# First attention in 32- and 64-row tiles on one Trainium2 core: row sums from a column of ones, division after the values

## The reference

```
attention: 8 heads of 64 channels, scores = q k^T / 8
  heads 0-3: query i sees keys i-31 .. i             (local)
  heads 4-7: query i sees keys j <= i with i % 32 == j % 32   (strided)
  attn = exp(scores - max) / (sum + 1e-9);  out = attn @ v
mixing: theta = x @ w_theta; zr, zi = x cos(theta), x sin(theta)
  y = w_tok_r @ zr + w_tok_i @ zi;  u = x + y;  u + relu(u @ w_ch)
experts: gate = softmax of the 2 largest of x @ w_gate (4 experts)
  each expert: causal attention with head size 64, times its gate, @ wo, summed
```

## Time and profile before

| | us |
|---|---|
| median of 3 runs | 575.8 |
| profiled execution, its own time | 575.45 |
| its span, first to last instruction | 573.7 |
| PE busy | 545.1 |
| DVE busy | 348.9 |
| ACT busy | 259.6 |

### The profile page before, as it was taken

How to read it: one execution, slowest core, us unless ns; L and a number is a source line. 1 busy time by engine, 2 the same in 40 slices (tenths; PEclk the granted TensorE clock), 3 DMA queues, 4 the chain that set the end, 5 groups by cost and what they waited for, 6 DMA issues and landing times.

```text
span 573.7 us, 11679 instructions
## 1 busy us (share of the span) xinstructions
PE 545.1 (95%) x4473; PEld 467.0 (81%) x4473; DVE 348.9 (61%) x843; ACT 259.6 (45%) x775; POOL 130.4 (23%) x131
## 2 busy tenths in 40 slices
PE   6999999999999999999999999999999999999986
PEld 5777889989866799899876689999976679998764
DVE  1677856675888622476678741567677952343683
ACT  2874734555533541355553542255643454121453
POOL 4550710022221250011321152011131126000110
PEclk9999999999999999999999999999999999999999
DMA  9742046221000114211000012331000010000002
GB/s 224 178 115 77 1 112 158 67 49 27 2 0 1 38 47 112 66 43 30 14 1 2 19 65 55 83 83 23 22 1 1 1 75 10 1 2 1 0 1 83
DMA packets 73413, 27.13 MB, mean 47 GB/s; under 512 B 68624, under 2 KB 68624, under 8 KB 73360
## 3 DMA queue, kind: packets, MB, share of 16 engines
q1 hardware_dynamic: 68848, 24.38, 16.7%
q10 hardware_dynamic: 4512, 2.02, 1.3%
HBM read 21.67 MB, written 4.72 MB: 46 GB/s over the span
## 4 chain that ended last, share of the span: by engine, by line
PE 74%; DVE 15%; ACT 5%; issue 3%; POOL 2%; POOLq 0%; DVEq 0%; ACTq 0%
PE acc L1278 33%; PE wide L1278 14%; PE wide L1350 4%; PE turned L1447 4%; PE turned L1391 3%; PE wide L1371 3%; PE turned L1404 2%; DVE xt L1106 2%; PE turned L1421 2%; DVE nmax L1049 2%; PE turned L1489 2%; PE turned L1311 2%; ACT probs L902 2%; PE wide L1335 1%; DVE probs L1080 1%
## 5 line engine op out<-in xcount | busy, mean ns | idle before, releaser
L814 POOL TENSOR_TENSOR probs<-probs,rec 96x768 f32<-96x768 f32 (+1 forms) x16 | 21.7, 1354 | 204.2 <-DVE rec L1064 204.2
L910 ACT ACTIVATE pt<-turned 128x384 f32<-128x384 f32 (+3 forms) x64 | 30.8, 481 | 77.4 <-PE turned L1404 41.4
L895 ACT ACTIVATE probs<-wide,nmax 96x128 f32<-96x128 f32 (+1 forms) x176 | 61.5, 369 | 9.0 <-DVE nmax L1045 8.9
L823 POOL TENSOR_TENSOR probs<-probs,weight 128x128 f32<-128x128 f32 (+4 forms) x36 | 26.9, 767 | 145.9 <-DVE weight L1087 145.9
L902 ACT ACTIVATE probs<-wide,nmax 128x128 f32<-128x128 f32 (+4 forms) x72 | 39.0, 553 | 36.2 <-DVE nmax L1049 25.6
L1278 PE MATMUL wide<-w_tok_hi,z_hi 128*128 128x288 f32 x216 | 47.4, 300 | 0.0
L1278 PE MATMUL wide<-w_tok_hi,z_lo 128*128 128x288 f32 x216 | 46.0, 293 | 0.0
L1278 PE MATMUL wide<-w_tok_lo,z_hi 128*128 128x288 f32 x216 | 45.9, 293 | 0.0
L1049 DVE TENSOR_REDUCE nmax<-wide 128x1 f32<-128x128 f32 (+4 forms) x72 | 33.1, 512 | 13.1 <-PE wide L1376 13.0
L840 POOL TENSOR_TENSOR z_lo<-absf,z_hi 128x512 fp32r<-128x512 f32 x20 | 26.3, 1317 | 63.9 <-ACT z_hi L958 63.9
L1278 PE MATMUL acc<-xu_hi,w_ch_hi 128*128 128x288 f32 x128 | 39.3, 307 | 1.0 <-DVE xu_lo L1176 0.9
(11 more groups left out here) (190 smaller groups left out, 1458.9 us busy)
## 6 DMA issues: line engine op xcount, KB each, us to landing
raw_q<-in_q SPq DMA_DIRECT2D x32, 128.0 KB, 2.4
out<-o_sb SPq DMA_DIRECT2D x16, 256.0 KB, 2.0
raw_k<-in_k SPq DMA_DIRECT2D x28, 128.0 KB, 2.5
raw_v<-in_v SPq DMA_DIRECT2D x64, 31.5 KB
raw_v<-in_v SPq DMA_DIRECT2D x14, 120.0 KB
raw_r<-in_moe_w_tok_r SPq DMA_DIRECT2D x1, 1152.0 KB, 6.3
stage<-in_moe_w_theta ACTq DMA_DIRECT2D x2, 512.0 KB, 7.5
raw_i<-in_moe_w_tok_i SPq DMA_DIRECT2D x1, 1024.0 KB, 7.9
```

The lines of the kernel that those rows point to most:

```text
L814: g.tensor_tensor(pr, pr, rec[0:rows, 1, 0:nt].unsqueeze(2).broadcast_to([rows, nt, w]), ALU.mult).then_inc(s["probs_pool"], 1)
L823: ins = g.tensor_tensor(pr, pr, weight[:, j:j + 1].broadcast_to([P, n]), ALU.mult)
L895: e = a.activation(probs[0:rows, hh, t * P:t * P + w], wide[slot][0:rows, t * P:t * P + w], ACT.Exp, bias=nmax[0:rows, hh, t:t + 1], accum ...
L910: ins = a.activation(dst, src, ACT.Copy)
```

## The change

The first attention (s1) is computed in small tiles. A local unit has 18 tiles of 32 queries by 64 keys (the 32 own keys and the 32 before them), a strided unit has 10 tiles of 3 classes (54 rows) and one of 2 (36). Four tiles of 32 rows, or two of 64, lie under each other on the partitions of PSUM, so one unit's scores fill one buffer of `wide`: one bank a head, 5 columns of 64 keys (local) or 6 (strided). The masks become one bf16 product a head; a small product with `never` closes the 32 keys before the first query.

The exponentials keep their number nearly (10 or 12 of 64 columns, in place of 12 or 10 of 126 and 128) and make no sums. One transpose takes both heads of a column (5 or 6 in place of 12 or 10). In `values` the transposed probabilities are the stationary operand, and v moves, with a column of ones added (65 columns): the result has queries on partitions, its 65th column is the row's sum. `norm` reads the sums there, and divides while it copies to `x_tok`. A new step `back` transposes `x_tok` (5 or 6 transposes) and `xt` is copied from that. POOL has no part in s1's `norm` any more; ACT makes the copies of both q and k. v is loaded in other pieces (6 DMAs a unit; for local heads each row twice), the masks are built after the semaphore that lets PE begin, and six products that nobody reads ("fill") stand first on PE.

`PROLOGUE` and `BODY` are now written out as lists of steps, in another order, s3, theta and out included. `EPILOGUE` is the same. The diff, cut to its core, with one line of the new lists:

```diff
-LQ = 96
-L_T = S // LQ
+W = 64
+L_T = S // STRIDE
 R_N = S // STRIDE
-R_T = P // R_N
+R_T = W // R_N
 SQ = R_T * R_N
 S_T = (STRIDE + R_T - 1) // R_T
-S_LAST = S - SQ * (S_T - 1)
+COLS = (S_T * W + P - 1) // P
+ZONE_A = 2 * (2 * NT + 6) * 2 * D + 2 * S + 36
+PROBS = 6 * P
+DV = D + 1
 MASKED = -1.0e30
...
+    ("exp", "s3", 0, 1, 1), ("scores", "s3", 1, 0), ("theta", 1, 0, 2), ("norm", "s3", 0, 1, 1), ("done", "theta", 0),
...
+    if k == "back":
+        return ["turned"] * 2
+    if k == "values" and step[1] == "s1":
+        return ["turned"] * 2 if step[4:] else ["wide"]
-        return ["wide"] * 2
+        return ["wide"] * (1 if step[1] == "s1" else 2)
...
-            return (LQ, L_T, P) if local(p) else (SQ, S_T, SQ)
+            return (STRIDE, L_T, STRIDE, L_T * STRIDE // P + 1) if local(p) else (W, S_T, SQ, COLS)
+        def parts(p):
+            return (0, 3), (3, tiles(p)[3])
+        def values_in(step, uses):
+            if step[4:]:
+                return [("turned", u, turned[u[0]]) for u in uses]
+            return [("wide", uses[0], wide[uses[0][0]][:, hh * 512:(hh + 1) * 512]) for hh in range(2)]
+        def place_of(uses, hh):
+            return uses[min(hh, len(uses) - 1)]
...
+            for hh in range(2):
+                if local(p):
+                    before_, own_ = [slice(hh * W + x * STRIDE, hh * W + (x + 1) * STRIDE) for x in range(2)]
+                    for dst, first, n in ((raw_v[before_, slot, 0:1, 0:D], 0, 1), (raw_v[own_, slot, :, 0:D], 0, L_T),
+                                          (raw_v[before_, slot, 1:L_T, 0:D], 0, L_T - 1)):
+                        eng.dma_start(dst, one[:, hh, first:first + n * STRIDE, :]
+                                     .rearrange("a (t p) d -> (a p) t d", p=STRIDE)).then_inc(s[f"v_loaded{slot}"], 16)
+                else:
+                    of = one[:, hh, :, :].rearrange("a (j r) d -> (a j) r d", r=STRIDE)
+                    for x in range(R_T):
+                        row = hh * W + x * R_N
+                        n = (STRIDE - x + R_T - 1) // R_T
+                        eng.dma_start(raw_v[row:row + R_N, slot, 0:n, 0:D], of[:, x:STRIDE:R_T, :])\
+                            .then_inc(s[f"v_loaded{slot}"], 16)
...
+                    for dst, use, scale in ((qt, u[0], SCALE), (kt, u[1], 1.0)):
+                        dst, src = turned_qk(dst, banks[where][use[0]][:, 0:NB], step[2], 0)
+                        wait_full(act, where, use)
+                        a.activation(dst, src, ACT.Copy, scale=scale).then_inc(read[where][use[0]], 1)
...
+                        for t in range(tiles(step[2])[3]):
+                            at0 = hh * 512 + t * W
+                            e = a.activation(tiled[:, t, hh * W:(hh + 1) * W], wide[slot][:, at0:at0 + W], ACT.Exp,
+                                             bias=nmax[:, hh, t:t + 1])
...
+                        cols = tiles(step[2])[3]
+                        places = note[("values", step[2])]
+                        heads = [slice(0, 2)] if len({u for _, u, _ in places}) == 1 else [slice(0, 1), slice(1, 2)]
+                        made = []
+                        for hs in heads:
+                            place, u, bank = places[hs.start]
+                            if place == "wide":
+                                of = wide[u[0]][:, :].rearrange("p (h n) -> p h n", h=2)
+                            else:
+                                of = bank[:, :].unsqueeze(1)
+                            made.append(of[:, :, 0:cols * DV].rearrange("p h (t n) -> p h t n", n=DV))
+                            wait_full(dve, place, u)
+                            v_.tensor_scalar(den[:, hs, 0:cols].unsqueeze(3), made[-1][:, :, :, D:DV], EPS, None, ALU.add)\
+                                .then_inc(s["den"], 1)
+                        dve.wait_ge(s["den"], c.at("den", len(heads)))
+                        v_.reciprocal(rec[:, :, 0:cols], den[:, :, 0:cols]).then_inc(s["recip"], 1)
+                        dve.wait_ge(s["recip"], c.at("recip", 1))
+                        for hs, of in zip(heads, made):
+                            place, u, _ = places[hs.start]
+                            to = x_tok[:, 0:cols, :].rearrange("p t (h n) -> p h t n", h=2)[:, hs, :, :]
+                            v_.tensor_tensor(to, of[:, :, :, 0:D],
+                                             rec[:, hs, 0:cols].unsqueeze(3).broadcast_to([P, len(range(2)[hs]), cols, D]),
+                                             ALU.mult).then_inc(read[place][u[0]], 1)
...
+                    copies, mask = (copies_l, mask_l) if local(p) else (copies_s, mask_s)
+                    for hh in range(2):
+                        mm(wide[slot][:, hh * 512:hh * 512 + cols * W], copies[:, :],
+                           mask[:, :].unsqueeze(1).broadcast_to([part, cols, W]), start=True, stop=True,
...
+                        n = min(rows, S - rows * t)
+                        q0 = rows * t
+                        k0 = max(q0 - STRIDE, 0) if local(p) else q0
+                        row, at0 = part * t % P, part * t // P * W + (STRIDE if local(p) and t == 0 else 0)
+                        for hh in range(2):
                             hd = slice(hh * D, (hh + 1) * D)
-                            ins = mm(wide[slot][0:n, t * P:t * P + k1 - k0], qt[hd, rows * t:rows * t + n],
-                                     kt[hd, k0:k1], start=False, stop=True, skip_group_check=True)
-                            if t == nt - 1:
-                                ins.then_inc(full["wide"][slot], 1)
+                            ins = mm(wide[slot][row:row + n, hh * 512 + at0:hh * 512 + at0 + q0 + n - k0],
...
+                        part, nt, _, cols = tiles(step[2])
+                        for n, (ca, cb) in enumerate(((0, 3), (3, cols))):
+                            slot = free("turned", n)
+                            if n == 0:
+                                u = note[("scores", step[2])]
+                                pe.wait_ge(read["wide"][u[0]], u[1])
+                            for t in range(ca, cb):
+                                k = min(P, part * nt - t * P)
+                                ins = nc.tensor.transpose(turned[slot][:, (t - ca) * P:(t - ca) * P + k],
+                                                          tiled[0:k, t, :], ident[0:k, 0:k])
                             ins.then_inc(full["turned"][slot], 1)
                     else:
...
+                    places = values_in(step, uses)
+                    for t in range(nt):
+                        keys = W if local(p) else min(rows, S - rows * t)
+                        row, at0 = part * t % P, part * t // P * DV
+                        for hh, (place, u, bank) in enumerate(places):
+                            ins = mm(bank[row:row + part, at0:at0 + DV],
+                                     tiled_t[hh * W:hh * W + keys, part * t:part * (t + 1)],
+                                     raw_v[hh * W:hh * W + keys, p % 2, t, :], start=True, stop=True)
+                            if t == nt - 1 and (place == "turned" or hh == 1):
+                                ins.then_inc(full[place][u[0]], 1)
...
+                elif kind == "back":
+                    p = step[2]
+                    part, nt = tiles(p)[0:2]
+                    for place, u, _ in note[("values", p)]:
+                        pe.wait_ge(read[place][u[0]], u[1])
+                    for n, (ca, cb) in enumerate(parts(p)):
+                        slot = free("turned", n)
+                        for t in range(ca, cb):
+                            k = min(P, part * nt - t * P)
+                            ins = nc.tensor.transpose(turned[slot][:, (t - ca) * P:(t - ca) * P + k], x_tok[0:k, t, :],
+                                                      ident[0:k, 0:k])
+                        ins.then_inc(full["turned"][slot], 1)
...
```

More of the change, by code:

```diff
@@ L348, in events @@
         return {"negmax": 1}
+    if k == "load":
+        return {"ones": 1}
+    if k == "norm" and step[1] == "s1":
+        return {"den": 2 if step[4:] else 1, "recip": 1}
     if k == "norm":
@@ L1095, in emit @@
                 elif kind == "values" and step[1] == "s1":
+                    note[("values", step[2])] = values_in(step, uses)
+                elif kind == "back":
                     p = step[2]
@@ L1327, in emit @@
                     p = step[2]
[L1328 to L1337 removed]
+                    part, nt, rows, cols = tiles(p)
@@ new lines, in emit @@
+                    for u in note[("turned", p)]:
+                        pe.wait_ge(read["turned"][u[0]], u[1])
+                    for n in range(len(uses)):
+                        free("turned" if step[4:] else "wide", n)
+                    places = values_in(step, uses)
[8 more added lines that the diff above has]
+                                ins.then_inc(full[place][u[0]], 1)
@@ new lines, in emit @@
```

(8 more changed lines are left out.)

451 lines of the change are left out of this document (163 added, 288 removed), and 17 rows, old and new, of the table BODY.

## The result

The changed kernel takes 560.95 us (median of 4 runs, 559.95 to 562.62) against 575.68 (575.46 to 576.6): ratio 0.9744, 95% interval 0.9715 to 0.9773. The forecast was 557. Its profiled execution has a span of 559.9 us and lasted 561.68, 13.8 us shorter in span than that of before.

A forecast was written before the change was run, and what follows sets the result against it. PE was taken to bound the bodies, by its own work and 3.7 us of waits; in the prologue PE and DVE alternate. From 575.45, -8.7 (work), -6.0 (waits) and -4.0 (prologue), plus the median's offset, gave 557; range 545 to 574.

The forecast's parts named there:

- PE's work in a body, -2.9: s1 on PE in each body: 14.2 us for four units against 17.1, so -8.7 us for three bodies.
- 14 ns a pass: s1's scores and values on PE: 464 passes a body at 14.4 ns, 6.7 us; bounded by 7 and 60 ns.
- Rival 2: Scores and values on PE: eight tiles overlap, 7 ns a pass in local units; 545 us with waits going too; chance 0.11.
- Waits in the bodies, -2.0 each: PE's nine waits in a body: 2.0 of 3.7 us go, -6.0 for three; bounds 0 and -11.
- Prologue, -4: Prologue and what follows up to the first body: steps (a) to (d) taken as -4 us, bounds 0 and -8.
- so nothing, and up to +1: v's more and smaller loads, behind theta's step: values stand 8 us or more later, so nothing; up to +1 in first unit.
- Step (a): Start of the prologue: PE's first instruction waits less for POOL's mask work, -2.0 us, with 0.5 as lower bound.
- (b): Prologue, first to last scores, three loops in 24.4 us: put at 0, bounds -3 and +3.
- (c): Prologue, last scores to theta: 9.4 us in place of 10.7, so -1.3.
- (d): Behind theta: `back` and `xu` of the last quarter +0.5; the `w_tok_lo` wait goes, -1.3 with the small ones.
- the -0.8: Forecast difference for the stretch from theta to the first body, -0.8 us.
- Exponentials at 0.22: ACT: s1's 44 exponentials without sums at 0.22 us each in place of 0.34, giving 5 us back.

The follow-up runs named there:

- both swaps: Changed kernel with the bodies' s3, theta and out in the order of before: 568.91 us; kernel before with the new order of these: 573.41 us.
- the run with w_theta later: Changed kernel with v of the second unit, w_tok and the second half of w_theta all loaded later in the prologue: 560.71 us, ratio 0.9753.
- the one with sums: Changed kernel with row sums made again by s1's exponentials (accum_out), read by nobody: 560.08 us, ratio 0.9743.

## Why the prediction was right, and where it was off

- *PE's work in a body, -2.9.* Measured -3.2. By its terms: a local unit is now turn 0.7, masks and `never` 0.4, scores 0.85, values 0.91, back 0.7 (134.73 to 135.46 in the timeline), 3.6 us; a strided one 3.5; 14.2 for four units, the sum of the forecast. Inside, two sizes were off against each other, which is luck: passes with filling took 6.6 and not 7.9, turn and back at 0.13 to 0.15 a transpose 6.1 and not 4.8. And of the 3.2 in busy time only 2.1 came with the tiles in the old order; 1.1 came with the new list.
- *14 ns a pass.* Right in kind, and shown: with two tiles the gain is gone. The rule of the Trainium skill ("TensorE: Matmul & The Clock Gate", section "Wait — 56ns, not 53.3ns?") that starts never follow each other by less than about 25 ns doesn't hold for passes in different tiles; the trace has 11.8 on average over 72. The Trainium skill ("TensorEngine Tiling (Array Packing)", section "Key Properties") says that different tiles run in parallel, and the trace agrees, for eight tiles too: 11.8 with eight at hand, against 14.4 with four. Rival 2 (7 ns) happened in part: a group of 72 takes 0.85 us, between the 1.2 that 14.4 ns and 0.15 for filling give and the 0.65 of 7 ns.
- *Waits in the bodies, -2.0 each.* Measured -2.0 in the first body, as the sum of +0.7 (the tiles in the old order) and -2.7 (the new list), which the forecast hadn't kept apart; that it met the number is in part luck. The reason was half right. The new order of s3 took the waits for `pt`, shown by both swaps; that it was the theta products between turn and values is the reading of the lists. That DVE and ACT do less was not the cause: with the old order and the new tiles the waits stay. That the longer way to `xt` makes waits of its own was named in the prediction and priced at nothing; the tiles by themselves lengthen the waits (3.7 to 4.4), which the new order has to pay back first. So the forecast's shares, 2.9 for the tiles and 2.0 for the waits, aren't what the runs give: 1.4 for the tiles alone, 3.4 to 3.8 for the list on top.
- *Prologue, -4: failed.* The step is the one that took v's pieces "so nothing, and up to +1". v of the local units is read twice, 208 KB more a unit, into queues that were already full to 15 us; PE, now faster through its first two units, reached transfers that hadn't landed. Two waits of 3.7 us together, and slower products behind them, took the -2.0 of the start, the -1.3 at the end, and 1.5 more. The slower products are 1.4 us behind the wait for k (21.85 to 25.34, 3.49 us, where the run with w_theta later has 2.10 for the same steps at full clock) and 1.6 behind the wait for v (38.66 to 47.20, 8.54 for 6.95). With the 3.7 that is 6.7 of the prologue up to theta, which came 4.8 later than forecast; so, as an estimate from these rows, the loops themselves gained some 2 us where the forecast had 0. The late rise of the clock at the start is in this execution too. The bounds of this term, 0 and -8, didn't hold the +1.5 of this execution; the one with sums, with the same loads, has -1.3. Step (a) was right (first scores at 8.45 for 8.4). In (b) the first to the last scores took 26.6 for 24.4, in (c) the last scores to theta 12.2 for 9.4. In (d) the wait for `w_tok_lo` went, as forecast, but from theta to the first body PE's busy time rose by 1.1 us (51.0 to 52.2; `back` is 0.85 of it), and nothing of the -0.8 was left.
- *Exponentials at 0.22.* Right (0.216). The 5 us of ACT that it gives back had no effect on the time that the run with sums could show.
- *The total.* 557 for 560.95: the bodies gave 0.6 more than forecast, the prologue and what follows it up to the first body, 4.6 less by the medians.

Open: how much of the prologue each of bytes, number of transfers, issue order and the clock at the start holds. Fewer bytes helped at one place and the total by 2.8 us of median, with intervals that overlap.

## What to carry to other kernels

Small products are cheap only while neighbours in the instruction stream lie in different tiles of the array: write the loops so that output group and head change from one product to the next, and price them by a row with as many tiles. A change that makes one stage faster should be checked against the transfers that feed it, and each transfer that is read again against how full the queues are there, by the DMA share of that stretch. Order and tile shape are one choice: the tiles alone gave 1.4 of the 5.1 us a body that both gave together. And before two prologues are compared, look where the clock of each is first recorded: two executions with the same loads were 1.6 us apart by 14 us for that alone.

## What the runs showed of the hardware

- fp32 passes of 64 columns: 11.8 ns on average with eight tiles taking turns, 14.4 with four, 20.8 with two; of 54 columns 16.1 with four and 24.8 to 25.9 with two (filling and ending of the group included). At 54 columns a set of passes, one in each tile, starts every 50 ns, whether there are two tiles or four.
- Row sums cost ACT 0.07 us an exponential of 64 columns, as an instruction of its own in the trace.
- Issuing six transfers of v took ACT 4.3 us (ACT's queue, 7.45 to 11.79) while the queues were full, and its exponentials waited behind them; nothing but the idle reason "issue" says so. In the run with sums the same six took 3.05.
- The first products of every kernel here run at half pace, up to the first record of the granted clock at 6.1 to 15.6 us; the clock column says 1.00 there without a record.
- Times of the changed kernel spread over 2.7 us, those of before over 1.1: granted clocks over the span between 0.994 and 0.997, and down to 0.985 in its relatives, against 0.999 to 1.000.
